# Two diagonal blocks in one visit: moving small matmuls together in TensorE's instruction stream

## The reference

```python
for t in range(S):
    kt, vt, bt = (k_n[:, :, t], v[:, :, t], beta[:, :, t, None])
    y[:, :, t] = np.einsum('bhd,bhde->bhe', q[:, :, t], state)
    v_old = np.einsum('bhde,bhd->bhe', state, kt)
    state = state + bt[:, :, :, None] * np.einsum('bhd,bhe->bhde', kt, vt - v_old)
...
h = x @ w_in
g = h * (1.0 / (1.0 + np.exp(-h)))
return (g @ w_out).astype(np.float32)
```

## Time and profile before

| | us |
|---|---|
| median of 3 runs | 836.79 (836.32 to 839.62) |
| the profiled execution | 835.71 |
| its span | 834.0 |
| TensorE matmul busy | 793.1 |
| VectorE busy | 569.0 |
| ScalarE busy | 369.1 |

### The profile page before, as it was taken

One profiled execution on the slowest core, in us unless ns is written; L12 is line 12 of the kernel. 1 busy time (PEld: TensorE's weight loads), 2 busy tenths in 40 slices (PEclk: granted clock), 3 DMA queues, 4 the chain that ended last, 5 costly groups with the idle time before them and its releaser, 6 DMA issues.

```text
span 834.0 us, 29247 instructions
## 1 busy us (share of the span) xinstructions
PE 793.1 (95%) x12158; PEld 724.2 (87%) x12159; DVE 569.0 (68%) x1504; ACT 369.1 (44%) x1042; POOL 112.6 (14%) x281
## 2 busy tenths in 40 slices
PE   5978999999999999999999999999999989999994
PEld 3557888899989999889999999999999989999993
DVE  6967887878578685777777677654323667767751
ACT  3722443434435353443434535343543556666641
POOL 1000000001010010101002010000103054344441
PEclk9989999999999999999999999999999999999998
DMA  8743112121211223112220211211023546655610
GB/s 271 219 160 123 46 53 66 60 89 48 92 48 40 91 65 97 42 50 87 66 91 22 66 47 66 64 41 47 32 86 118 186 133 208 198 191 184 188 32 14
DMA packets 46649, 79.75 MB, mean 96 GB/s; under 512 B 5680, under 2 KB 35082, under 8 KB 46144
## 3 DMA queue, kind: packets, MB, share of 16 engines
q1 hardware_dynamic: 43104, 73.07, 27.1%
q0 software_dynamic: 3424, 4.93, 1.9%
HBM read 67.05 MB, written 13.19 MB: 96 GB/s over the span
## 4 chain that ended last, share of the span: by engine, by line
issue 79%; POOL 9%; DMA 6%; POOLq 2%; PE 2%; DVE 1%; ACT 0%; SPq 0%
DMA id_table<-token,slot 5%; POOL idle L680 3%; POOL kq_t L735 2%; POOL id_table L725 2%; PE psum L980 1%; POOL ids_all L731 1%; DMA id_table<-x_sb 1%; POOL out L790 1%; DMA kd<-kq 1%; POOLq L509 0%; POOLq L510 0%; PE psum L836 0%; POOLq L757 0%; POOL token L718 0%; PE psum L981 0%
## 5 line engine op out<-in xcount | busy, mean ns | idle before, releaser
L1014 PE MATMUL psum<-xt_hi,w_hi 128*128 128x256 f32 x768 | 226.3, 295 | 5.3 <-issue 2.7
L1015 PE MATMUL psum<-xt_lo,w_hi 128*128 128x256 f32 x768 | 217.5, 283 | 0.0
L1016 PE MATMUL psum<-xt_hi,w_lo 128*128 128x256 f32 x768 | 217.2, 283 | 0.0
L1190 ACT ACTIVATE h_raw<-psum 128x256 f32<-128x256 f32 x192 | 73.6, 384 | 311.0 <-PE psum L1016 309.3
L1449 DVE TENSOR_TENSOR h_lo<-h_raw,h_hi 128x256 fp32r<-128x256 f32 x192 | 81.4, 424 | 160.2 <-ACT h_hi L1191 159.4
L1014 PEld LDWEIGHTS psum<-xt_hi,w_hi 128*128 128x128 f32 x768 | 145.3, 189 | 14.5 <-issue 8.8
L1016 PEld LDWEIGHTS psum<-xt_hi,w_lo 128*128 128x128 f32 x768 | 146.3, 190 | 0.0
L1015 PEld LDWEIGHTS psum<-xt_lo,w_hi 128*128 128x128 f32 x768 | 145.8, 190 | 0.0
L1038 PE MATMUL psum<-w_hi,h_hi 128*128 128x394 f32 x384 | 138.6, 361 | 1.1 <-DVE h_lo L1449 1.1
L1040 PE MATMUL psum<-w_hi,h_lo 128*128 128x394 f32 x384 | 131.2, 342 | 0.0
L1039 PE MATMUL psum<-w_lo,h_hi 128*128 128x394 f32 x384 | 131.0, 341 | 0.0
(11 more groups left out here) (183 smaller groups left out, 1121.8 us busy)
## 6 DMA issues: line engine op xcount, KB each, us to landing
kq_t<-kq SPq DMA_DIRECT2D x24, 512.0 KB, 3.6
bp<-moe_w SPq DMA_DIRECT2D x24, 512.0 KB, 4.5
kv_t<-kv SPq DMA_DIRECT2D x24, 384.0 KB, 3.1
bp<-moe_w SPq DMA_DIRECT2D x24, 384.0 KB, 4.2
kd<-kq SPq DMA_DIRECT2D x20, 256.0 KB, 3.3
x_table<-x_sb SPq DMA_DIRECT2D x13, 392.0 KB, 2.8
out<-x_sb SPq DMA_DIRECT2D x12, 384.0 KB, 3.1
bp<-moe_w_in SPq DMA_DIRECT2D x6, 512.0 KB, 6.0
```

The lines of the kernel that those rows point to most:

```text
L1014: m(out, hi, x_hi, start=first, stop=False)
L1015: m(out, hi, x_lo, start=False, stop=False)
L1016: return m(out, lo, x_hi, start=False, stop=last)
L1190: a_.activation(h_raw[i % 2][:, :], up_ps[i % 2][:, 0:G2], ACT.Silu)
```

## The change

At four places (odd pairs, slots 18 and 19) and four more (even pairs from the second, slots 0 and 1) the two steps' diagonal blocks were made in two slots, with an `up` in between, and evicted in the second. Now both are made and evicted in the first slot, right behind the carry or the read.

```diff
@@ -447,16 +447,16 @@
-                    if p % 2 and x in (18, 19) and g + 2 < NQ:
-                        s["diag"](g + 2, x - 18)
-                        if x == 19:
-                            for e in range(2):
-                                s["evict"](g + 2, 0, e)
-                    if p % 2 == 0 and p and x in (0, 1) and g + 1 < NQ:
-                        s["diag"](g + 1, 2 + x)
-                        if x == 1:
-                            for e in range(2):
-                                s["evict"](g + 1, 1, e)
+                    if p % 2 and x == 18 and g + 2 < NQ:
+                        for n in range(2):
+                            s["diag"](g + 2, n)
+                        for e in range(2):
+                            s["evict"](g + 2, 0, e)
+                    if p % 2 == 0 and p and x == 0 and g + 1 < NQ:
+                        for n in range(2, 4):
+                            s["diag"](g + 1, n)
+                        for e in range(2):
+                            s["evict"](g + 1, 1, e)
```

## The result

The change made the kernel slower: 839.88 us median of 20 runs (837.46 to 843.53) against 836.56 of 20 runs of before, a ratio of 1.0039 with a 95% interval of 1.0026 to 1.0052, or +3.3 us. The profiled execution took 839.33 us.

A forecast was written before the change was run, and what follows sets the result against it. TensorE, busy 793.1 of 834.0 us, was taken as the bound. Visit terms 0.89 + 0.94 + 0.91 + 0.18 - 0.10 - 0.54 gave +2.3 us, forecast 838.8 us, 8 in 10 range 834.8 to 841.8.

The forecast's parts named there:

- The mechanism: TensorE's stream: 256-instruction blocks, each ready some 3 us after the one before is entered; small matmuls use one up in 1.4.
- K1: First diagonal-block visit, behind the carry of pair 1: break 2 pairs before the end of the second half, +0.89 us.
- K2: Second visit, at the read of pair 2: break 31 pairs into the second half, +0.94 us.
- K4: Fourth visit, at the read of pair 4: break 59 pairs into the second half, +0.91 us.
- B: Second half of a visit, the second step's diagonal block: 64 pairs of weight load and matmul, 0.69 us.
- A: First half of a visit, the first step's diagonal block; 64 pairs, 0.69 us.
- K7: Seventh visit, behind the carry of pair 7: taken as -0.1 us, between -0.18 and +0.9.
- The first term, the changeover: Entering and leaving runs of small matmuls: merging saves 0.18 us per undisturbed visit, 1.4 us over eight.
- The second term: Instruction supply at visits: merged blocks no longer hide part of the fetch; +0.89, +0.94 and +0.91 us in three broken visits.
- K8: Eighth visit, at the read of pair 8: block end 3 or 4 pairs into the second half, +0.18 us.
- VectorE's queue: Evictions behind a carry: VectorE waits up to 1.8 us, costed at nothing; as rival +6.2 us, chance 0.10.
- The rival with the opposite sign: At all visits: breaks no fixed supply limit; changeovers alone -1.4 us, -3.1 if breaks vanish; chance 0.15.

The follow-up runs named there:

- The shifts: Unchanged and changed order with doubled or added matmuls that move the ends of 256-instruction blocks; ratios to the unchanged kernel 0.9968 to 1.0059.
- long_run: Changed kernel with one solve's 8 matmuls in pair 10 issued 64 times over, 2016 instructions more; 863.41 us in its one run.
- late: Against the unchanged kernel, both diagonal blocks made in the second slot, behind the up products; ratio 0.9982 (0.9960 to 1.0003), repeated 0.9974.
- after_again: The changed kernel profiled once more, nothing altered; 837.88 us, one execution of the unchanged kernel beside it 836.78.
- after_shift2: Changed order with doubled matmuls so that no block end falls in a visit, no small matmuls in the last stage; 834.37 us, 0.9968 to the unchanged kernel.
- before_shift2: Unchanged order with doubled matmuls so that no block end falls in a visit, no small matmuls in the last stage; 837.74 us, 0.9999 to the unchanged kernel.
- read_only: Changed kernel with the carry visits put back, so only the four visits at a read are merged; ratio to the unchanged kernel 1.0043.
- before_shift: Unchanged order with 512 added instructions, 208 of them small ones ahead of the last stage's warm-up; 839.47 us, ratio to the unchanged kernel 1.0059.
- after_p156: Changed kernel with 39 matmuls of the first pair's solves issued twice, 156 instructions; ratio to the unchanged kernel 1.0014.
- carry_only: Changed kernel with the read visits put back, so only the four visits behind a carry are merged; ratio to the unchanged kernel 1.0021.

## Why the prediction was right, point by point

- **The mechanism**: right. Breaks after 126, 95 and 123 pairs in K1, K2 and K4, where it put them "2 pairs before the end of B", "33 pairs of the read, 64 of A, then 31 of B" and "5, 64, then 59 of B". The shifts and `long_run` tell it from the rivals, and `late` shows that large matmuls ahead of the run cover the wait. One part of it does not hold everywhere: "A block seems to be asked for when the one before it has been entered". In K7 of after the packet came 1.1 us before that, and the supply from entry to going on was 1.7 us, not 3. The sentence of the Trainium skill ("Runtime: NRT & Kernel Launch", "Instruction fetch mechanics") that the fetch is hidden since the sequencer dispatches more slowly does not hold for small matmuls here: at 10 ns a pair a block lasts 1.3 us, and in `long_run`, at 12 ns a pair and 1.6 us a block, the next is there after 3.5 to 3.7 us. Its blocks of 256 instructions and its fetch of one page while the current one runs are what `long_run` shows. The prediction's 264 records per packet is only near 256: with waits and the rest TensorE has 24,828 instructions, 97 blocks for 92 packets, and no run here shows how the first five come.
- **The first term, the changeover**: mis-sized. It said that merging "saves 0.18 us in an undisturbed visit"; it saves 0.33 (2.60 for 2.93). The 0.69 us that I gave each half contained a changeover itself: the merged 128 pairs take 1.25 us to the next up product, not 1.38.
- **The second term**: near. K1, K2 and K4 cost +1.13, +0.74 and +1.13 where +0.89, +0.94 and +0.91 stood: 3.00 against 2.74. K8 -0.01 for +0.18, K7 +0.02 for -0.10; both had their break and gave it back in the larger changeover saving. In after_again K8 was 4.02 us, with 1.42 us from matmul to matmul at its break.
- **The sum**: +2.3 predicted, +2.05 in the visits of the profile, +3.3 in the median. That the first two lie so near is in part luck: the broken visits cost 0.26 more than the sum had, the three unbroken ones saved 0.42 more, and K7 and K8 came out 0.06 lower.
- **What was left out**: "TensorE is the bound for the whole stretch at full granted clock" was true of before only. The longer breaks brought half clock behind K1 in both profiles of the changed kernel, 1.5 us in the first. With the 2.05 of the visits that makes 3.6 of the 3.7 us between the two spans. The median is 1.1 us above the forecast of 838.8, and this is the likely reason; what share of the unprofiled executions had such a stretch no run shows.
- **VectorE's queue**: "up to 1.8 us in K1" was 0.4, since its subtraction of the carry ended late itself, and nothing reached TensorE.
- **The rival with the opposite sign** (changeovers alone, -1.4 us) holds where no block end falls into a visit, as `after_shift2` against `before_shift2` shows.

Why breaks of the same visit differ by up to 1 us from execution to execution (K8: 0.38 us from matmul to matmul in after, 1.39 in read_only) is settled in part: in read_only K8's packet started 0.4 us later behind the block's first instruction and took 1.36 us instead of 0.93. What stays open is why packets start and last as they do, and what the 1.5 us behind K8 were; there TensorE waited 2.2 us for a gather of rows in after and not in before, but 1.2 in before_shift too, which has the order of before.

## What to carry to other kernels

A run of small matmuls of over 100 pairs can be bound by instruction supply, and whether it is depends on where 256-instruction boundaries fall; so an edit of the order can gain or lose by its alignment alone, and should be timed at two alignments before it is judged. Put large matmuls ahead of such a run, inside the same 256 instructions, not behind it: in K1 of `late` 0.29 us of idle time stood where after had 2.01. Idle time of TensorE that no engine explains, at distances of whole multiples of 256 instructions, is the sign to look for.

## What the runs showed of the hardware that I had not expected

- Sustained supply of TensorE's instructions: 256 per 3.47 to 3.75 us (long_run), 3.47 us at either level of the clock. TensorE went on 1.2 to 1.6 us after the end of the last q8 packet at all 37 breaks seen, in nine profiles.
- Half clock followed 2.01, 2.05, 1.90, 1.90 and 1.76 us of idle time in diagonal blocks (K1 of after, after_again and long_run, K4 of read_only, K8 of after_p156) but not 1.94 us in carry_only, nor the 1.63 and 1.49 us of K4 and K2 in after. The length alone does not tell: ahead of an up product (L1014) near 674 us TensorE was idle for 2.7 to 2.8 us in before and in after alike, and only before went to half clock there.
- Weight load and matmul of 128 x 32 with 32 columns on one and the same tile took 33 ns a pair (before_shift), of 128 x 32 with 48 columns on changing tiles 15, of 64 x 32 on changing tiles about 10.
